# The row limits of two score tiles made in one VectorE operation instead of two

## The chip, the cores and the metric

The kernel runs on one core of a Trainium2 chip. The metric is the device time of one execution in microseconds (us). The core has TensorE (PE: matmuls, transposes), VectorE (DVE), ScalarE (ACT), GpSimd (POOL) and SyncE (SP, which issues the loads and moves here). Each engine works through its own queue in order; they meet at semaphores. TensorE's granted clock is 1.00 of its full level throughout.

## The reference

Attention over 4 batches of 8 heads with 576 rows and 64 features, followed by two MLP layers over 2304 tokens, all fp32. The part around the change:

```python
scores = scale * np.matmul(q, k.transpose(0, 1, 3, 2))
thresh = np.max(scores, axis=-1, keepdims=True) - tau
scores = np.where(scores >= thresh, scores, -1000000000.0)
scores = scores - np.max(scores, axis=-1, keepdims=True)
attn = np.exp(scores)
attn = attn / (np.sum(attn, axis=-1, keepdims=True) + 1e-09)
return np.matmul(attn, v).astype(np.float32)
...
h = x @ w_in
r = np.maximum(h, 0.0)
g = s * (r * r) + b
return (g @ w_out).astype(np.float32)
...
h = x @ w_in
g = h * (1.0 / (1.0 + np.exp(-1.702 * h)))
return (g @ w_out).astype(np.float32)
```

## The kernel before

The attention is cut into 160 tiles of 96 or 128 query rows by 576 keys. Two tiles, j even and j odd, make a beat; there are 80 beats with tiles and a few behind them. Matmul operands are split into a high and a low part of a narrower format (`_hi`, `_lo`, `q_hl`); ScalarE makes the high parts, GpSimd most of the low ones by a subtraction.

A tile goes through these steps. TensorE computes its scores into one of two PSUM tensors (`scores[j % 2]`). DVE's `row_max(j)` (L1045) multiplies them by the negative scale in place and writes the row's minimum, the negated maximum, to column `j % 8` of `neg_max`; this form comes as two instructions, the main one and a read of the accumulator (`DVE_READ_ACCUMULATOR`). ScalarE takes the exponent into `prob` (L1269). `limit_of(j)` (L1052) adds tau to that column of `neg_max` and writes the column of `limit`. `mask(j)` (L1071) zeroes what lies beyond the limit and sums the row. GpSimd adds epsilon to the two sums of a beat (L1547); `invert_pair` (L1059) on DVE takes their reciprocals in the next beat; GpSimd's norm (L1554) scales both tiles. TensorE and ScalarE turn the tiles of the first groups over, DVE (L1085) with moves by SyncE those of the later ones, and TensorE multiplies with the values: a context piece. ScalarE and DVE (`act_lo`, L1093) split a piece into high and low for the layers.

From beat 15 on (`MLP_FROM`) each beat also carries one step `s = beat - 15` of the first layer: on TensorE `output` of step s - 3 and `hidden` of step s, on ScalarE the relu, on DVE `gated(s - 1)` (L1101) and `gated_lo(s - 2)` (L1108, the tile `g_lo`), on GpSimd the low parts of two weight slabs (L1560, L1567). GpSimd's splits of a query tile (L1532) and a key tile (L1540) fall in the beats in which one is due.

The order on every engine is written out by hand in that engine's block. DVE's beat is: maximum and limit of the even tile, piece, reciprocals, gated, maximum and limit of the odd tile, mask of the even tile, g_lo, mask of the odd tile, piece, transposes. DVE's semaphore `max_ready` counts maxima, `limit_ready` limits. Before a tile's scores are overwritten, TensorE waits for the mask of the tile two before (`masked`).

Of the kernel before, what the change touches and what calls it, by code (L numbers as in the profile page):

```python
# [9 lines left out]
ALU = mybir.AluOpType  # L10
# [45 lines left out]
TILES = FIRST_TILE[-1]  # L56
# [11 lines left out]
def rows_of(j):  # L68
    return ROWS[GROUPS_OF[TILE_AT[j][0]][3]]
# [245 lines left out]
def tiles_of(beat, lag=0):  # L315
    return range(2 * beat - lag, 2 * beat - lag + 2)
# [41 lines left out]
def build(nc, q, k, v, consts_in, ident_in, slabs, twin_in, twin_out, out):  # L358
    ctx = ExitStack()
    with ctx:  # L360
# [7 lines left out]
        tau_in, s_c, b_c, eps_c, scale_c, tau_c, lower_c = (consts[:, n:n + 1] for n in range(7))  # L368
# [68 lines left out]
        neg_max = sbuf(attn, "neg_max", [P, STATS])  # L437
        limit = sbuf(attn, "limit", [P, STATS])
# [44 lines left out]
        max_ready = sem("max_ready")  # L483
        exp_ready = sem("exp_ready")
        limit_ready = sem("limit_ready")
# [532 lines left out]
        def _(dve):  # L1018
# [27 lines left out]
                                        accum_out=neg_max[0:m, j % STATS:j % STATS + 1]  # L1046
                                        ).then_inc(max_ready, 1)

            def limit_of(j):
                m, r = rows_of(j), j % STATS  # L1050
                dve.wait_ge(max_ready, j + 1)
                nc.vector.tensor_scalar(limit[0:m, r:r + 1], neg_max[0:m, r:r + 1], tau_c[0:m, :], None, ALU.add  # L1052
                                        ).then_inc(limit_ready, 1)

            def invert_pair(j):
# [5 lines left out]
            def mask(j):  # L1061

                m, r = rows_of(j), j % STATS
                dve.wait_ge(limit_ready, j + 1)
                dve.wait_ge(exp_ready, j + 1)
                if j % 2 == 1 and riding(j // 2) is not None:
                    dve.wait_ge(context_hi_ready, riding(j // 2) + 1)
                if j % 2 == 0 and turn_due(j // 2 - MLP_FROM) is not None:
                    dve.wait_ge(x_ready, turns_by(j // 2 - MLP_FROM))
                p = prob[0:m, j % PROBS, :].rearrange("p (a n) -> p a n", a=2)  # L1070
                nc.vector.scalar_tensor_tensor(  # L1071
                    out=p, in0=scores[j % 2][0:m, :, 0:HALF], scalar=limit[0:m, r:r + 1],
                    in1=p, op0=ALU.is_le, op1=ALU.mult,
                    accum_out=row_sum[0:m, r:r + 1]).then_inc(masked, 1)
# [22 lines left out]
            def gated(n):  # L1097

                dve.wait_ge(gate_ready, n + 1)
                g = gate[:, n % 2, :]  # L1100
                nc.vector.scalar_tensor_tensor(out=g, in0=h_bank(n)[:, 0:TOK], scalar=s_c, in1=g, op0=ALU.mult,  # L1101
                                               op1=ALU.mult).then_inc(square_ready, 1)
# [80 lines left out]
            for beat in range(BEATS):  # L1183
                s = beat - MLP_FROM
                for j in tiles_of(beat):
                    if j < TILES:
                        row_max(j)
                        limit_of(j)
                    if j % 2 == 0 and alone(beat - 1) is not None:
                        context_lo(alone(beat - 1))  # L1190
                    if j % 2 == 0 and 0 <= j - 2 < TILES:
                        invert_pair(j - 2)
                    if j % 2 == 0 and s >= 1:
                        gated(s - 1)
                for j in tiles_of(beat):
                    if j < TILES:
                        mask(j)
                    if j % 2 == 0 and s >= 2:
                        gated_lo(s - 2)
                if riding(beat) is not None:  # L1200
                    context_lo(riding(beat))
                for j in tiles_of(beat, 2):
                    if PE_TILES <= j < TILES:
                        turn(j)
# [497 lines left out]
```

## Time and profile before

| | |
|---|---|
| median of 3 runs | 1011.58 us (1011.28 to 1013.16) |
| the profiled execution | 1009.4 us, of which the span of the trace is 1007.6 us |
| TensorE busy | 993.2 us, 99% of the span |
| VectorE busy | 798.0 us, 79%, 1749 instructions |
| GpSimd busy | 657.9 us, 65% |
| ScalarE busy | 606.6 us, 60% |
| granted clock of TensorE | 1.00 |

Busy time counts an instruction from its start to the end that the profiler gives it; on TensorE the ends are modelled, and neighbours overlap, so 99% is not a peak rate. In a timeline an instruction's start is the more exact figure, and the step from start to start tells what an instruction cost its engine. DVE's busy time is spread unevenly: the attention ends at about 490 us.

### The profile page before, as it was taken

Reading aid. Unit: us, or ns where it says so; the run is one execution under the profiler, and the core shown is the slowest. Engines: PE = TensorE matmul, PEld = TensorE weight load, DVE = VectorE, ACT = ScalarE, POOL = GpSimd, SP = SyncE. Lnnn points to the kernel's source line nnn. Section 1 sums busy time; section 2 is a strip of 40 time slices with the busy share of each in tenths; the row PEclk is TensorE's granted clock in tenths of the full one; section 3 lists DMA queues with packets and bytes.
Section 4 is the critical chain, followed back from the end, with each engine's and each line's share of the span. In section 5 each row is a group of like instructions: output and inputs, shape, how many; then the busy total and the mean of one; then the engine's idle time right before and its main releaser. Section 6 shows DMA issues by size and latency. Waiting matters only on the chain.

```text
span 1007.6 us, 18212 instructions
## 1 busy us (share of the span) xinstructions
PE 993.2 (99%) x5922; PEld 895.4 (89%) x5922; DVE 798.0 (79%) x1749; ACT 606.6 (60%) x1124; POOL 657.9 (65%) x713
## 2 busy tenths in 40 slices
PE   8999999999999999999999999999999999999998
PEld 7788888888888888888899999998989989899897
DVE  7989999999999999999547766877767776566663
ACT  7877666666676666765555755555546555454443
POOL 6769997778788888886657775454544545445452
PEclk9999999999999999999999999999999999999999
DMA  7236776897977797778733541112122221222212
GB/s 216 73 116 187 209 204 189 218 239 213 228 199 191 204 246 190 209 179 217 211 106 126 185 150 32 63 42 85 44 82 87 102 84 46 81 87 102 84 48 79
DMA packets 97581, 142.50 MB, mean 141 GB/s; under 512 B 10320, under 2 KB 68944, under 8 KB 97488
## 3 DMA queue, kind: packets, MB, share of 16 engines
q1 hardware_dynamic: 97488, 141.34, 48.7%
q8 instruction: 49, 0.80, 0.3%
q14 instruction: 44, 0.36, 0.1%
HBM read 102.96 MB, written 4.72 MB: 107 GB/s over the span
## 4 chain that ended last, share of the span: by engine, by line
PE 85%; DVE 11%; issue 1%; DMA 1%; ACT 1%; POOL 0%; SPq 0%; DVEq 0%; POOLq 0%; ACTq 0%
PE shared L831 12%; PE y_ps L850 11%; PE shared L924 10%; PE y_ps L948 10%; PE scores L948 10%; PE scores L924 8%; PE scores L745 7%; PE scores L807 7%; PE scores L831 5%; PE y_ps L870 5%; DVE scores L1045 4%; DVE prob L1071 3%; PE scores L870 2%; DVE blocks L1085 1%; DMA k_raw<-k 1%
## 5 line engine op out<-in xcount | busy, mean ns | idle before, releaser
L1269 ACT ACTIVATE prob<-scores,neg_max 128x576 f32<-128x576 f32 (+1 forms) x160 | 118.6, 742 | 122.5 <-DVE scores L1045 122.4
L1614 POOL TENSOR_TENSOR a_sum_lo<-a_sum,a_hi 128x256 fp32r<-128x256 f32 x96 | 70.1, 740 | 182.5 <-DVE scores L1167 123.9
L1560 POOL TENSOR_TENSOR w_lo<-w_raw,win_hi 128x512 fp32r<-128x512 f32 x96 | 129.1, 1345 | 22.1 <-ACT win_hi L1311 17.7
L1567 POOL TENSOR_TENSOR w_lo<-w_raw,wout_hi 128x512 fp32r<-128x512 f32 x96 | 126.5, 1318 | 23.4 <-ACT wout_hi L1318 23.4
L1045 DVE TENSOR_SCALAR_CACHE_REDUCE scores<-scores,consts 128x576 f32<-128x576 f32 (+1 forms) x160 | 129.5, 809 | 13.1 <-PE scores L745 11.7
L1554 POOL TENSOR_SCALAR prob<-prob,row_inv 128x576 f32<-128x576 f32 (+1 forms) x160 | 126.8, 805 | 6.1 <-DVE row_inv L1059 5.7
L1071 DVE SCALAR_TENSOR_TENSOR prob<-scores,limit,prob 128x576 f32<-128x576 f32 (+1 forms) x160 | 128.1, 808 | 0.3
L831 PE MATMUL shared<-act_hi,win_hi 128*128 128x384 f32 x280 | 94.8, 339 | 1.1 <-DVE gate L1101 0.9
L831 PE MATMUL shared<-act_hi,w_lo 128*128 128x384 f32 x280 | 94.3, 337 | 0.0
L831 PE MATMUL shared<-act_lo,win_hi 128*128 128x384 f32 x280 | 93.9, 335 | 0.0
L1085 DVE STREAM_TRANSPOSE blocks<-prob 128x576 f32<-128x576 f32 (+1 forms) x128 | 91.4, 751 | 1.9 <-DMA prob_t<-blocks 1.7
L1108 DVE SCALAR_TENSOR_TENSOR g_lo<-gate,consts,g_hi 128x384 fp32r<-128x384 f32 x96 | 92.7, 966 | 0.2 <-ACT g_hi L1332 0.2
L1179 DVE TENSOR_TENSOR g_lo<-gate,g_hi 128x384 fp32r<-128x384 f32 x96 | 62.2, 650 | 33.4 <-ACT g_hi L1403 32.8
L745 PE MATMUL scores<-k_hi,q_hl 128*128 128x288 f32 (+1 forms) x320 | 76.6, 320 | 6.8 <-DVE prob L1071 6.2
L1332 ACT ACTIVATE g_hi<-gate,consts 128x384 fp32r<-128x384 f32 x96 | 59.0, 614 | 38.8 <-PE y_ps L870 27.9
L1395 ACT ACTIVATE gate<-scores 128x384 f32<-128x384 f32 x48 | 23.6, 492 | 94.9 <-DVE scores L1167 94.9
L1403 ACT CAST g_hi<-gate 128x384 fp32r<-128x384 f32 x96 | 49.2, 514 | 49.4 <-DVE gate L1174 40.0
L850 PE MATMUL y_ps<-wout_hi,g_hi 128*128 128x512 f32 x192 | 75.6, 394 | 0.0
L850 PE MATMUL y_ps<-wout_hi,g_lo 128*128 128x512 f32 x192 | 75.5, 393 | 0.0
L807 PE MATMUL scores<-prob_t,v_sb 128*64 128x192 f32 x800 | 73.8, 331 | 1.5 <-DVE prob L1071 0.9
L850 PE MATMUL y_ps<-w_lo,g_hi 128*128 128x512 f32 x192 | 74.9, 390 | 0.0
L1532 POOL TENSOR_TENSOR q_hl<-q_raw,q_hl 128x384 fp32r<-128x384 f32 (+1 forms) x51 | 49.0, 961 | 37.7 <-DVE g_lo L1108 31.2
(157 smaller groups left out, 2956.6 us busy)
## 6 DMA issues: line engine op xcount, KB each, us to landing
w_raw<-slabs SPq DMA_DIRECT2D x93, 512.0 KB, 4.2
a_raw<-twin_in SPq DMA_DIRECT2D x24, 512.0 KB, 4.6
o_raw<-twin_out SPq DMA_DIRECT2D x24, 512.0 KB, 3.6
prob_t<-blocks SPq DMA_DIRECT2D x96, 120.0 KB, 2.8
k_raw<-k SPq DMA_DIRECT2D x32, 288.0 KB, 4.6
prob_t<-blocks SPq DMA_DIRECT2D x96, 96.0 KB, 2.9
v_sb<-v SPq DMA_DIRECT2D x26, 320.0 KB, 4.3
q_raw<-q SPq DMA_DIRECT2D x40, 192.0 KB, 4.4
```

The lines of the kernel that those rows point to most:

```text
L745: mm = nc.tensor.matmul(scores[j % 2][0:m, half, 0:HALF], q_hl[i % Q_RING][:, q0:q0 + m], part[key_slot(e)][:, half * HALF:(half + 1) * HALF],
L807: mm = nc.tensor.matmul(place, v_sb[:, i % 2, side, c, :], rows, start=(c == 0), stop=(c == KEY_CHUNKS - 1))
L831: mm = nc.tensor.matmul(bank[:, 0:TOK], wp[:, w], act_at(xp, c, tile * TOK, TOK), start=(c == 0 and k == 0), stop=(c == DC - 1 and k == 2))
L850: mm = nc.tensor.matmul(y_ps[g][:], gp[:, n % 2, toks], wp[:, :], start=(f == 0 and k == 0), stop=(f == SLABS - 1 and k == 2))
L924: mm = nc.tensor.matmul(twin_bank(x), wp, xp, start=(c == 0 and k == 0), stop=(c == 1 and k == 2))
L948: mm = nc.tensor.matmul(z_bank(tile, g), gp[:, i, toks], wp, start=(e == 0 and i < 2 and k == 0), stop=(e == TWIN_SLABS - 1 and i >= 2 and ...
L1045: nc.vector.tensor_scalar(place, place, scale_c[0:m, :], None, ALU.mult, ALU.min, accum_out=neg_max[0:m, j % STATS:j % STATS + 1]).then_in ...
L1071: nc.vector.scalar_tensor_tensor(out=p, in0=scores[j % 2][0:m, :, 0:HALF], scalar=limit[0:m, r:r + 1], in1=p, op0=ALU.is_le, op1=ALU.mult, ...
L1269: nc.scalar.activation(prob[0:m, j % PROBS, :].rearrange("p (a n) -> p a n", a=2), scores[j % 2][0:m, :, 0:HALF], ACT.Exp, bias=neg_max[0: ...
L1554: nc.gpsimd.tensor_scalar(prob[0:m, j % PROBS, :], prob[0:m, j % PROBS, :], row_inv[0:m, r:r + 1], 1.0, ALU.mult, ALU.mult).then_inc(norme ...
L1560: nc.gpsimd.tensor_tensor(in_of(w_lo, n), in_of(w_raw, n), win_hi[n % IN_HI][:].bitcast(F32), ALU.subtract).then_inc(win_lo_ready, 1)
L1567: nc.gpsimd.tensor_tensor(out_of(w_lo, n), out_of(w_raw, n), wout_hi[n % OUT_HI][:].bitcast(F32), ALU.subtract).then_inc(wout_lo_ready, 1)
```

## The change

The limits of a beat's two tiles are no longer made one by one, each behind its own maximum. One operation with two columns makes both, behind the second maximum and ahead of the first mask. It waits for both maxima and counts `limit_ready` up by one for the two tiles; `mask` waits for the beat's count.

```diff
-            def limit_of(j):
+            def limit_pair(j):
+
                 m, r = rows_of(j), j % STATS
-                dve.wait_ge(max_ready, j + 1)
-                nc.vector.tensor_scalar(limit[0:m, r:r + 1], neg_max[0:m, r:r + 1], tau_c[0:m, :], None, ALU.add
+                dve.wait_ge(max_ready, j + 2)
+                nc.vector.tensor_scalar(limit[0:m, r:r + 2], neg_max[0:m, r:r + 2], tau_c[0:m, :], None, ALU.add
                                         ).then_inc(limit_ready, 1)
...
             def mask(j):
 
                 m, r = rows_of(j), j % STATS
-                dve.wait_ge(limit_ready, j + 1)
+                dve.wait_ge(limit_ready, j // 2 + 1)
                 dve.wait_ge(exp_ready, j + 1)
...
                 for j in tiles_of(beat):
                     if j < TILES:
                         row_max(j)
-                        limit_of(j)
                     if j % 2 == 0 and alone(beat - 1) is not None:
                         context_lo(alone(beat - 1))
                     if j % 2 == 0 and 0 <= j - 2 < TILES:
                         invert_pair(j - 2)
                     if j % 2 == 0 and s >= 1:
                         gated(s - 1)
+                if 2 * beat < TILES:
+                    limit_pair(2 * beat)
                 for j in tiles_of(beat):
                     if j < TILES:
                         mask(j)
```

No other engine's sequence changes. On VectorE, in a beat ahead of the first layer (a beat of 96-row tiles; scores0 and scores1 are the tensors of the even and the odd tile), the rows before are

```order
L1045 TENSOR_SCALAR scores0,neg_max<-scores0,consts 96x2x288 [waits scores_ready]
L1052 TENSOR_SCALAR limit<-neg_max,consts 96x1 [waits max_ready]
L1093 TENSOR_TENSOR act_lo0<-shared,act_hi0 128x128 [waits context_hi_ready]
L1059 RECIPROCAL row_inv<-row_sum_eps 128x2 [waits sum_eps_ready]
L1045 TENSOR_SCALAR scores1,neg_max<-scores1,consts 96x2x288 [waits scores_ready]
L1052 TENSOR_SCALAR limit<-neg_max,consts 96x1 [waits max_ready]
L1071 SCALAR_TENSOR_TENSOR prob,row_sum<-scores0,limit,prob 96x576 [waits exp_ready,limit_ready]
```

and of the changed kernel, same engine and place:

```order
L1045 TENSOR_SCALAR scores0,neg_max<-scores0,consts 96x2x288 [waits scores_ready]
L1094 TENSOR_TENSOR act_lo0<-shared,act_hi0 128x128 [waits context_hi_ready]
L1060 RECIPROCAL row_inv<-row_sum_eps 128x2 [waits sum_eps_ready]
L1045 TENSOR_SCALAR scores1,neg_max<-scores1,consts 96x2x288 [waits scores_ready]
L1053 TENSOR_SCALAR limit<-neg_max,consts 96x2 [waits max_ready]
L1072 SCALAR_TENSOR_TENSOR prob,row_sum<-scores0,limit,prob 96x576 [waits exp_ready,limit_ready]
```

The first limit is gone, the second has two columns, and the first mask needs the result of the operation directly ahead of it. (From L1053 on the changed kernel's lines have numbers higher by one.)

On VectorE in a beat with a layer step, where `gated` (gate<-shared) stands between the two maxima, the rows before are

```order
L1045 TENSOR_SCALAR scores0,neg_max<-scores0,consts 96x2x288
L1052 TENSOR_SCALAR limit<-neg_max,consts 96x1
L1059 RECIPROCAL row_inv<-row_sum_eps 128x2
L1101 SCALAR_TENSOR_TENSOR gate<-shared,consts,gate 128x384
L1045 TENSOR_SCALAR scores1,neg_max<-scores1,consts 96x2x288
```

and of the changed kernel:

```order
L1045 TENSOR_SCALAR scores0,neg_max<-scores0,consts 96x2x288
L1060 RECIPROCAL row_inv<-row_sum_eps 128x2
L1102 SCALAR_TENSOR_TENSOR gate<-shared,consts,gate 128x384
L1045 TENSOR_SCALAR scores1,neg_max<-scores1,consts 96x2x288
L1053 TENSOR_SCALAR limit<-neg_max,consts 96x2
```

The reciprocals and `gated` come directly behind the first maximum.

## Rows read from the trace of the kernel before

**Rows 1.** The page's part 1, busy time, share and instructions by engine.

```profile
PE 993.2 (99%) x5922; PEld 895.4 (89%) x5922; DVE 798.0 (79%) x1749; ACT 606.6 (60%) x1124; POOL 657.9 (65%) x713
```

**Rows 2.** Three stretches: length, busy PE, PEld, DVE, ACT, POOL; clock, DMA share, GB/s.

```profile
10.00:66.00 56.00, 49.79 (x496) 43.49 (x496) 52.83 (x164) 46.80 (x96) 41.30 (x61) 1.00 0.36 112
66.00:132.00 66.00, 63.44 (x406) 55.88 (x404) 63.31 (x164) 48.28 (x94) 60.65 (x66) 1.00 0.66 195
132.00:484.00 352.00, 351.40 (x2262) 309.43 (x2261) 337.23 (x846) 230.92 (x432) 284.37 (x322) 1.00 0.80 209
```

**Rows 3.** Waits of DVE from 132 to 484 us: total, times, longest.

```profile
DVE scores L1045 <- PE scores L745: 8.8, 19, 1.1
DVE blocks L1085 <- DMA prob_t<-blocks: 1.7, 3, 0.9
```

**Rows 4.** The chain that ended last, in beat 9: start, us, what.

```profile
43.90 0.21 DVE limit L1052
...
46.21 0.81 PE scores L745 x4
```

**Rows 5.** Timeline of DVE, beat 9: start us, us, instruction, idle before.

```profile
42.98 0.83 DVE L1045 TENSOR_SCALAR_CACHE_REDUCE scores<-scores,consts 128x576 f32<-128x576 f32 x1 [0.15 <-PE scores L745]
43.72 0.14 DVE L1045 DVE_READ_ACCUMULATOR scores<-scores,consts 128x1 f32 x1
43.90 0.21 DVE L1052 TENSOR_SCALAR limit<-neg_max,consts 128x1 f32<-128x1 f32 x1
44.03 0.28 DVE L1093 TENSOR_TENSOR act_lo<-shared,act_hi 128x128 fp32r<-128x128 f32 x1
44.23 0.15 DVE L1059 RECIPROCAL row_inv<-row_sum_eps 128x2 f32<-128x2 f32 x1
...
45.20 0.21 DVE L1052 TENSOR_SCALAR limit<-neg_max,consts 128x1 f32<-128x1 f32 x1
45.34 0.81 DVE L1071 SCALAR_TENSOR_TENSOR prob<-scores,limit,prob 128x576 f32<-128x576 f32 x1
46.07 0.08 DVE L1071 DVE_READ_ACCUMULATOR prob<-scores,limit,prob 128x1 f32 x1
46.07 0.81 DVE L1071 SCALAR_TENSOR_TENSOR prob<-scores,limit,prob 128x576 f32<-128x576 f32 x1
```

**Rows 6.** Timeline of DVE, three of the second layer's weight sums.

```profile
591.27 0.41 DVE L1149 TENSOR_TENSOR a_sum<-a_raw 128x256 f32<-128x256 f32 x1
591.60 0.41 DVE L1151 TENSOR_TENSOR a_sum<-a_raw,a_sum 128x256 f32<-128x256 f32 x1
592.05 1.41 DVE L1154 TENSOR_TENSOR a_sum<-a_raw,a_sum 128x256 f32<-128x256 f32 x1
```

**Rows 7.** Three lines of DVE: duration in ns, least/median/greatest; first and last start.

```profile
L1052 DVE TENSOR_SCALAR limit<-neg_max,consts x160: 208/214/217, 7.9 to 481.2; 128x1 f32<-128x1 f32 x96, 96x1 f32<-96x1 f32 x64
...
L1059 DVE RECIPROCAL row_inv<-row_sum_eps x80: 119/154/158, 11.8 to 484.9; 128x2 f32<-128x2 f32 x80
...
L1108 DVE SCALAR_TENSOR_TENSOR g_lo<-gate,consts,g_hi x96: 607/617/1728, 81.0 to 627.4; 128x384 fp32r<-128x384 f32 x96
```

**Rows 8.** Timeline of POOL in beats 2, 9, 10 and 22.

```profile
16.41 1.40 POOL L1540 TENSOR_TENSOR k_lo<-k_raw,k_hi 128x576 fp32r<-128x576 f32 x1
...
44.48 1.47 POOL L1554 TENSOR_SCALAR prob<-prob,row_inv 128x576 f32<-128x576 f32 x2 [0.41 <-DVE row_inv L1059]
...
48.54 1.47 POOL L1554 TENSOR_SCALAR prob<-prob,row_inv 128x576 f32<-128x576 f32 x2
...
110.63 1.78 POOL L1554 TENSOR_SCALAR prob<-prob,row_inv 96x576 f32<-96x576 f32 x2
```

**Rows 9.** Timeline of DVE: the second limit in beats 2, 10 and 22.

```profile
16.88 0.21 DVE L1052 TENSOR_SCALAR limit<-neg_max,consts 128x1 f32<-128x1 f32 x1
...
49.26 0.21 DVE L1052 TENSOR_SCALAR limit<-neg_max,consts 128x1 f32<-128x1 f32 x1
...
111.02 0.21 DVE L1052 TENSOR_SCALAR limit<-neg_max,consts 96x1 f32<-96x1 f32 x1
```

## The prediction

> **What bounds the kernel now.** I read the page's busy shares first: TensorE (PE) is busy 993.2 us of the 1007.6 us span, VectorE (DVE) 798.0 [rows 1]. An average over stages says little, so next came the busy time by stretch. The reader is to see three regimes in it [rows 2]. In 10 to 66 us (attention alone, beats 1 to 14) DVE is busy 52.8 of 56 us and PE 49.8. In 66 to 132 us (the first layer joins) DVE has 63.3 of 66, PE 63.4, GpSimd (POOL) 60.7. In 132 to 484 us PE has 351.4 of 352 and DVE 337.2. Third, the waits of DVE in that last stretch: 8.8 us for PE's scores and 1.7 us for a move, 10.5 us in 54 beats [rows 3]. So DVE sets the pace up to about 132 us, and behind that PE does, with DVE some 0.2 us a beat from setting it.
>
> The chain shows the loop of an early beat: first limit 0.21 us, and at the end the first mask's result lets PE compute the next scores, 0.81 us [rows 4], which the next first maximum waits for. The two maxima, the limits and the first mask are all inside; only the second mask lies beside the scores. What a beat saves or loses ahead of its first mask is therefore lost or won in full up to 66 us.
>
> **The change, step by step.** All steps below are start-to-start times of one early beat [rows 5].
>
> Removed: the first limit and its wait. The first maximum's accumulator read starts at 43.72, the limit that waits for it at 43.90 (0.18), and the next instruction, which waits for neither, at 44.03 (0.13). Where nothing waits on an accumulator read, the next instruction starts with it: behind the first mask, read and second mask both start at 46.07. Taking that for the maximum too, act_lo starts at 43.72 instead of 44.03: 0.31 us less. Bounds: if the maximum's read of 0.14 us can't be overlapped, 0.17 is left.
>
> Added: the first mask now waits for an operation that stands directly before it. At 45.20 the limit starts and the mask follows at 45.34, since it waits only for the limit of long before. The nearest rows are three sums: the second (591.60) starts 0.33 behind its predecessor, whose result it doesn't need, and the third, which waits for the second, 0.45 behind that one [rows 6]. So a wait on the predecessor costs 0.12. I take 0.12, bounds 0.05 (the mask's issue hides a part) and 0.18 (the step from read to limit). Second column: reciprocal with two columns is shorter than limit with one, 154 against 214 ns [rows 7], so I give it nothing. Net so far: 0.31 less, 0.12 more, 0.19 us a beat less, between 0 and 0.26.
>
> On that price the Trainium skill says otherwise: "VectorE: DVE Perf Modes", section "The DRAIN you can't avoid", has a chain of Vector operations take the same time with a semaphore behind each as with one at the end, and advises fewer operations, not fewer waits. By that rule only the limit's own step of 0.13 would be saved and no 0.12 added, 0.13 a beat less instead of 0.19. Rows 5 and 6 disagree with it: the waits there cost 0.18 and 0.12.
>
> The term that decides is what the new operation meets. In the old form limit lasts 208 to 217 ns in all 160 cases though GpSimd is nearly always at work; reciprocal is as constant; but g_lo lasts from 607 to 1728 ns, by what GpSimd runs beside it [rows 7]. So there are DVE operations that GpSimd's hold up, for up to 1.1 us, and others that it doesn't. A tensor-with-scalar operation from SBUF to SBUF that is more than one column wide has no row in this trace. Bounds: nothing, as for one column, or the rest of the GpSimd instruction in progress. I take the second, by choice: the two free rows are one of the old width and one of another operation.
>
> The Trainium skill is what tips me. "SBUF — State Buffer", section "Who interferes with whom", has tensor_scalar (not the form with an accumulator) enter modes that use both port pairs, and then it and GpSimd exclude each other for a whole instruction; "Vector Engine (DVE) Microarchitecture Reference", section 5.1, has fp32 with two elements per partition do so. g_lo in rows 7 agrees in kind; the two-column limit no run here shows.
>
> Price of it: the pair arrives where the second limit starts now, less 0.31. Let POOL's instruction in progress run to its end, and add 0.1 for handing over (of the size of the 0.12 above). Beats 1 to 14 fall in three kinds.
> - Six (1, 5, 8, 9, 11, 13): the norms are released by reciprocal and move with it. The first norm (44.48, now 44.17, 0.74 long) ends at 44.91, and the pair comes at 44.89 [rows 5, 8]. Wait 0.02, net 0.17 less: together 1.0 less.
> - Three (10, 12, 14): a wider q split ahead keeps the norms back. Norm from 48.54 to 49.28, pair at 48.95 [rows 8, 9]. Wait 0.43, net 0.24 more: 0.7 more.
> - Five (2, 3, 4, 6, 7): the 1.40 us split of a key runs. In beat 2 it lasts from 16.41 to 17.8, and the pair comes at 16.57 [rows 8, 9]: 1.3. The five waits read 1.3, 1.0, 0.6, 0.6, 0.6, sum 4.2, less 5 x 0.19: 3.2 more.
>
> Sum to 66 us: 2.9 us slower. Beats 15 and 16 wait for the first matmuls of the layer and count nothing. Beats 17 to 25 read the same way give waits from 0 to 0.76 (beat 22: norm from 110.63, pair at 110.71 instead of 111.02, 0.65 and 0.1 [rows 8, 9]), in sum 4.3, less 9 x 0.19: 2.6 slower; POOL, as full as DVE there, can't give it back. Beats 26 to 79: waits 22.7 us in 54 beats, less 54 x 0.19: 12.4 us more on DVE, against 10.5 us that it waits now. PE hides most; about 1 us is left. What is late next, if the cover is gone, is the masks: behind the pair stand both masks, g_lo and the transposes, and PE's next scores wait for the masks. Bounds: 0 and, with half a wait more in each beat, 6.
>
> Sum: 2.9 + 2.6 + 1 = 6.5 us. The profiled execution took 1009.4 us, so 1015.9 by its measure; the median of the three runs is 2.2 us above it. Forecast: 1018.0 us.
>
> **The rivals.**
> - *Held by nothing, faster.* The pair starts at once beside any GpSimd instruction, as limit and reciprocal do [rows 7]. Then 14 x 0.19 = 2.7 us up to 66 us. From 66 to 132 us DVE would save 9 x 0.19 = 1.7, but PE idles only 2.6 us there [rows 2] and POOL is near full; I give 1.0. Behind that PE is the bound: 0. Together 3.7: 1007.9 us. For it: 160 steady limits. Against it: nothing but the width. It decides once the mean wait is under 0.19 us a beat.
> - *The accumulator read isn't overlapped.* The saving is 0.17, the new wait 0.12 to 0.18: 0.05 or 0 a beat, at most 14 x 0.05 = 0.7 us: 1011.3 us. For it: the maximum's read lasts 0.14, the mask's 0.08. Against it: the mask's read is wholly overlapped.
> - *Held, but the wait falls away.* The key splits are fed by ScalarE and the masks of the beat before, so that the beat could settle with the pair between two instructions, as six beats do already: waits of 0.2 a beat on average, no difference: 1011.6 us. Against it: the two instructions that follow on POOL stand in its queue with no gap.
>
> **How the numbers follow.** Chances: forecast mechanism 0.60 (nearly all of it slower), held by nothing 0.25, read not overlapped 0.07, wait falls away 0.08. A measurement of this kernel tells about 0.2%, 2.0 us. Slower: 0.60 less 0.04 for a size under 2 us = 0.56; faster: 0.25 less 0.03 = 0.22; the rest, 0.22, within. The range starts below the rival's 1007.9, since it holds a quarter, at 1007.2 and ends at 1022.0, where late beats leak 4 to 5 us instead of 1. The forecast's own range is 1014 to 1022.
>
> **What would show it.** Right: the new limit lasts from 0.21 up to 1.5 us, or the gap behind the maximum's read grows, case by case with POOL's instruction; 80 of them hold 20 to 35 us; the norms in turn stretch; the beats of the first kind shrink by 0.1 to 0.2 us, and the ones with a key split grow by 0.4 or more. DVE's wait for PE in 132 to 484 us goes towards 0. The step maximum to act_lo is 0.74 instead of 1.05, and pair to mask 0.25 where POOL is idle. Wrong: 80 limits of 0.21 to 0.22 us. Then the first rival holds, and every early beat shrinks by 0.19 us; if its act_lo starts 0.14 later than the read, the second.

## The result and the profile of the changed kernel

The changed kernel takes 1019.03 us in the median of six runs (1017.29 to 1020.27), the kernel before 1010.63 us in six (1009.16 to 1013.16). The ratio is 1.0088, with a 95% interval of 1.0076 to 1.0099: slower by 0.9%. The profiled execution of the changed kernel took 1018.54 us, its span is 1016.7 us, 9.1 us more than before.

The page's part 1 of the changed kernel, which answers to [rows 1]:

```profile
span 1016.7 us, 18132 instructions
PE 994.8 (98%) x5922; PEld 895.9 (88%) x5922; DVE 805.0 (79%) x1669; ACT 609.4 (60%) x1124; POOL 655.7 (64%) x713
```

DVE has 80 instructions fewer and is busy 7.0 us longer. The same three stretches as in [rows 2]:

```profile
10.00:66.00 56.00, 46.80 (x454) 41.45 (x456) 51.62 (x138) 43.09 (x87) 38.48 (x57) 0.97 0.35 108
66.00:132.00 66.00, 62.23 (x418) 53.72 (x415) 63.32 (x152) 48.85 (x95) 56.81 (x64) 1.00 0.64 186
132.00:484.00 352.00, 348.77 (x2236) 307.09 (x2235) 336.35 (x787) 231.22 (x430) 284.15 (x321) 1.00 0.78 206
```

PE does 3.0 us less of its work up to 66 us, 1.2 less up to 132 and 2.6 less up to 484, so all three stretches lose.

Two lines of DVE, durations in ns least/median/greatest, against [rows 7]. First the new limit:

```profile
L1053 DVE TENSOR_SCALAR limit<-neg_max,consts x80: 223/555/830, 8.9 to 489.7; 128x2 f32<-128x2 f32 x48, 96x2 f32<-96x2 f32 x32
...
L1060 DVE RECIPROCAL row_inv<-row_sum_eps x80: 119/158/168, 11.6 to 494.0; 128x2 f32<-128x2 f32 x80
```

The old limit took 208 to 217 ns in 160 cases. The new one takes from 223 to 830 ns. By its two shapes, busy time and mean of one:

```profile
L1053 DVE TENSOR_SCALAR limit<-neg_max,consts 128x2 f32<-128x2 f32 x48 | 22.8, 475 | 1.7
...
L1053 DVE TENSOR_SCALAR limit<-neg_max,consts 96x2 f32<-96x2 f32 x32 | 17.9, 559 | 1.1
```

That is 40.7 us in all; 80 free ones of 0.225 us would be 18.0. So they take 22.7 us more than free ones would. This is what being held means below; 62 of the 80 last over 0.24 us. The reciprocal, of two columns as well, stays nearly as it was (158 ns in the middle, 154 before).

What holds it is seen where the timelines of DVE and of POOL are laid side by side. DVE in beat 9, against [rows 5]:

```profile
45.87 0.83 DVE L1045 TENSOR_SCALAR_CACHE_REDUCE scores<-scores,consts 128x576 f32<-128x576 f32 x1 [0.15 <-PE scores L745]
46.61 0.14 DVE L1045 DVE_READ_ACCUMULATOR scores<-scores,consts 128x1 f32 x1
46.61 0.29 DVE L1094 TENSOR_TENSOR act_lo<-shared,act_hi 128x128 fp32r<-128x128 f32 x1
46.82 0.15 DVE L1060 RECIPROCAL row_inv<-row_sum_eps 128x2 f32<-128x2 f32 x1
46.95 0.83 DVE L1045 TENSOR_SCALAR_CACHE_REDUCE scores<-scores,consts 128x576 f32<-128x576 f32 x1
47.69 0.14 DVE L1045 DVE_READ_ACCUMULATOR scores<-scores,consts 128x1 f32 x1
47.87 0.69 DVE L1053 TENSOR_SCALAR limit<-neg_max,consts 128x2 f32<-128x2 f32 x1
48.60 0.82 DVE L1072 SCALAR_TENSOR_TENSOR prob<-scores,limit,prob 128x576 f32<-128x576 f32 x1
```

And POOL, against [rows 8]:

```profile
47.07 1.47 POOL L1556 TENSOR_SCALAR prob<-prob,row_inv 128x576 f32<-128x576 f32 x2 [0.39 <-DVE row_inv L1060]
```

The two norms run from 47.07 to 48.54, so the second starts at 47.80. The limit is issued at 47.87, into that second norm, and ends at 48.56, 0.02 us behind it. In this trace 61 of the 62 end 0.02 to 0.03 us behind the end of a GpSimd instruction (norm L1556, k_lo L1542 or w_lo L1569); the other one, in beat 30, lasts only 0.25 us.

That also gives the price. A pair (the new limit of two columns) that starts with the time t to go in GpSimd's instruction lasts t + 0.02 us where t is over 0.2, and 0.23 us where it is less: its own 0.23 us run beside the wait and not behind it. So it costs t less 0.2. Beat 7 lies close to that limit: the pair starts 0.25 us before the end of a key split and lasts 0.27 us, hardly more than a free one. DVE first, then POOL:

```profile
39.41 0.27 DVE L1053 TENSOR_SCALAR limit<-neg_max,consts 128x2 f32<-128x2 f32 x1
...
38.24 1.41 POOL L1542 TENSOR_TENSOR k_lo<-k_raw,k_hi 128x576 fp32r<-128x576 f32 x1
```

All 56 pairs with more than 0.25 us to go follow this. Of the pairs that come within 0.04 us of the end of one instruction, those of beats 1 and 14 are free, and those of beats 21, 24, 42 and 75 are held to the end of the next (0.75 to 0.79 us).

From the first maximum to the first mask beat 9 took 2.36 us before (42.98 to 45.34 in [rows 5]) and takes 2.73 now. The beat grew nearly as much, from 4.06 to 4.45 us. This step from first maximum to first mask, called the **head** of a beat below, is the number by which the experiments are compared; all heads are of beat 8 or 9, which are alike in each kernel.

DVE's waits from 132 to 484 us, against [rows 3]; the wait for the move is gone, the one for PE is not:

```profile
DVE scores L1045 <- PE scores L745: 11.4, 19, 1.1
```

The chain that ended last, shares by engine: PE holds 76% (85% before), DVE 16% (11%).

```profile
PE 76%; DVE 16%; DMA 3%; issue 2%; ACT 2%; SPq 1%; POOL 0%; DVEq 0%; POOLq 0%; ACTq 0%
```

GpSimd has 0% in it. It has no share, although the experiments below show that it causes the delay: no semaphore joins it to the limit, and a held instruction shows up as a long instruction of the engine that is held.

### The profile page after: what moved, and what is told of

The parts are those of the page before. It is cut to its first block, busy times and chain, and to the rows that moved or that the text cites. A ratio compares the mean times of both kernels' runs of the same rounds, so it can differ in the third digit from the quotient of the medians.

```text
span 1016.7 us, 18132 instructions
## 1 busy us (share of the span) xinstructions
PE 994.8 (98%) x5922; PEld 895.9 (88%) x5922; DVE 805.0 (79%) x1669; ACT 609.4 (60%) x1124; POOL 655.7 (64%) x713
## 4 chain that ended last, share of the span: by engine, by line
PE 76%; DVE 16%; DMA 3%; issue 2%; ACT 2%; SPq 1%; POOL 0%; DVEq 0%; POOLq 0%; ACTq 0%
PE shared L924 10%; PE scores L948 10%; PE y_ps L948 10%; PE shared L831 8%; PE scores L924 8%; PE y_ps L850 7%; PE scores L807 6%; DVE scores L1045 5%; PE scores L745 5%; PE scores L831 5%; PE y_ps L870 5%; DVE prob L1072 3%; DVE blocks L1086 3%; DVE g_lo L1109 2%; PE scores L870 2%
## 5 line engine op out<-in xcount | busy, mean ns | idle before, releaser
L1569 POOL TENSOR_TENSOR w_lo<-w_raw,wout_hi 128x512 fp32r<-128x512 f32 x96 | 126.5, 1318 | 23.5 <-ACT wout_hi L1320 23.5
L1556 POOL TENSOR_SCALAR prob<-prob,row_inv 128x576 f32<-128x576 f32 (+1 forms) x160 | 124.9, 794 | 3.6 <-DVE row_inv L1060 3.3
L1109 DVE SCALAR_TENSOR_TENSOR g_lo<-gate,consts,g_hi 128x384 fp32r<-128x384 f32 x96 | 88.7, 924 | 0.2 <-ACT g_hi L1334 0.2
L807 PE MATMUL scores<-prob_t,v_sb 128*64 128x192 f32 x800 | 73.8, 331 | 4.4 <-DVE prob L1072 4.3
```

The source lines that it names most:

```text
L807: mm = nc.tensor.matmul(place, v_sb[:, i % 2, side, c, :], rows, start=(c == 0), stop=(c == KEY_CHUNKS - 1))
L1556: nc.gpsimd.tensor_scalar(prob[0:m, j % PROBS, :], prob[0:m, j % PROBS, :], row_inv[0:m, r:r + 1], 1.0, ALU.mult, ALU.mult).then_inc(norme ...
L1569: nc.gpsimd.tensor_tensor(out_of(w_lo, n), out_of(w_raw, n), wout_hi[n % OUT_HI][:].bitcast(F32), ALU.subtract).then_inc(wout_lo_ready, 1)
```

## The experiments

Each edit is against the kernel before or the changed kernel, as said. The ratio is to the kernel before, run beside it (medians from 1010.14 to 1010.53 us), with its 95% interval. The theory under test: two columns make the limit wait out GpSimd's instruction in progress. The rivals: the loss is the new wait of the mask on its predecessor, or the order alone.

### The order alone, with narrow limits

From the kernel before: both limits behind the second maximum, each of one column.

```diff
                         row_max(j)
-                        limit_of(j)
...
                 for j in tiles_of(beat):
+                    if j < TILES:
+                        limit_of(j)
+                for j in tiles_of(beat):
                     if j < TILES:
                         mask(j)
```

> The order of the change without its width: both limits one column wide, directly behind each other after the second maximum. Theory (the two-column form is held by GpSimd's instructions): all 160 limits last 0.21 to 0.22 us, none follows GpSimd. The first beats save the first limit's wait (0.18 us) and nothing else; the second mask's wait lies behind the first mask: 14 x 0.18 = 2.5 us up to 66 us, about 1 us behind that, so 3 us faster than before (ratio 0.997). Rival (the order is what costs: the masks come later because the limits stand together): about as slow as the change, ratio 1.006 to 1.009.

Measured: 1005.56 us, ratio 0.9960 (0.9945 to 0.9974): faster. DVE in beat 9; x2 is the two limits together:

```profile
42.21 0.83 DVE L1045 TENSOR_SCALAR_CACHE_REDUCE scores<-scores,consts 128x576 f32<-128x576 f32 x1 [0.16 <-PE scores L745]
...
44.02 0.14 DVE L1045 DVE_READ_ACCUMULATOR scores<-scores,consts 128x1 f32 x1
44.02 0.39 DVE L1052 TENSOR_SCALAR limit<-neg_max,consts 128x1 f32<-128x1 f32 x2
44.33 0.81 DVE L1071 SCALAR_TENSOR_TENSOR prob<-scores,limit,prob 128x576 f32<-128x576 f32 x1
```

And all 160 limits, durations in ns as above:

```profile
L1052 DVE TENSOR_SCALAR limit<-neg_max,consts x160: 197/210/216, 8.8 to 476.7; 128x1 f32<-128x1 f32 x96, 96x1 f32<-96x1 f32 x64
```

The head is 2.12 us, 0.24 less than before, and no limit is held, though they stand in the place of the pair and 96 of the 160 start with more than 0.25 us to go in a GpSimd instruction. The first limit starts together with the second maximum's read, since it needs only the first maximum, and the first mask needs only the first limit. So the rival of the order is refuted: the place isn't what costs, and with two narrow limits it is a gain.

### The wait alone

From the kernel before: the mask of the even tile also waits for the odd tile's limit, which stands directly ahead of it.

```diff
-                dve.wait_ge(limit_ready, j + 1)
+                dve.wait_ge(limit_ready, j - j % 2 + 2)
```

> The order and both one-column limits of before; only the masks wait for both limits of their beat, so that the first mask waits for the operation directly before it. It prices the wait that the change adds. Both theories: pair-to-mask step 0.24 to 0.26 instead of 0.14 us, 14 x 0.12 = 1.7 us more up to 66 us and up to 9 x 0.12 = 1 us more from 66 to 132 us; ratio 1.001 to 1.003. If the wait is the main cost of the change, the ratio is 1.006 or more.

Measured: 1013.32 us, ratio 1.0031 (1.0018 to 1.0044).

```profile
46.17 0.21 DVE L1052 TENSOR_SCALAR limit<-neg_max,consts 128x1 f32<-128x1 f32 x1
46.42 0.82 DVE L1071 SCALAR_TENSOR_TENSOR prob<-scores,limit,prob 128x576 f32<-128x576 f32 x1
```

The step from limit to mask is 0.25 us, against 0.14 in [rows 5]; the head grows from 2.36 to 2.47 and the early beats from 4.05 to 4.18. So the wait costs 0.11 us an early beat here, and in all about a third of what the change lost.

The Trainium skill, "VectorE: DVE Perf Modes", "The DRAIN you can't avoid", has a chain of eight copies take the same time with a semaphore behind each as with one at the end. This run weighs against carrying that over to this kernel: the wait is the only edit, and the time moved.

### The width alone, on top of the wait

From the kernel with the wait alone: the odd tile's limit writes both columns. Even tiles keep their own narrow limit, so the count of instructions, the order and the waits don't change.

```diff
+                first = r - j % 2
-                nc.vector.tensor_scalar(limit[0:m, r:r + 1], neg_max[0:m, r:r + 1], tau_c[0:m, :], None, ALU.add
+                nc.vector.tensor_scalar(limit[0:m, first:r + 1], neg_max[0:m, first:r + 1], tau_c[0:m, :], None, ALU.add
```

> As the run with the wait alone, and the second limit of a beat makes both columns again, two wide; the first limit stays. The two kernels differ in the width of 80 operations. Theory (held by width): the 80 wide limits last 0.22 to 1.5 us by what GpSimd runs, the 80 narrow ones 0.21; slower than the change itself, since the first limit and its wait are still there: ratio 1.010 to 1.020. Rival (width costs nothing): the same as the run with the wait alone.

Measured: 1020.46 us, ratio 1.0110 (1.0094 to 1.0127). Wide and narrow limits of the one kernel, busy time and mean of one:

```profile
L1053 DVE TENSOR_SCALAR limit<-neg_max,consts 128x2 f32<-128x2 f32 x48 | 17.8, 371 | 1.7
...
L1053 DVE TENSOR_SCALAR limit<-neg_max,consts 96x2 f32<-96x2 f32 x32 | 13.8, 431 | 1.1
...
L1053 DVE TENSOR_SCALAR limit<-neg_max,consts 128x1 f32<-128x1 f32 x48 | 10.3, 214 | 1.7
...
L1053 DVE TENSOR_SCALAR limit<-neg_max,consts 96x1 f32<-96x1 f32 x32 | 6.7, 209 | 1.1
```

This is the cleanest pair: 80 operations are one column wider, and the median is 7.1 us longer (1020.46 less 1013.32). The granted clock doesn't explain it: the mean of an execution is 0.997 or 0.998 in three of the four with the wide limit, but the fourth, at 1.000, still took 1019.89 us. Where it costs differs from the changed kernel. Here nearly all the early beats are free (4.20 us, against 4.18 with the wait alone): in beat 9 the reciprocal starts at 46.07 and the wide limit at 47.04, 0.97 behind it, and the first norm runs from 46.32 to 47.06, so the limit finds 0.02 us to go and lasts 0.23. Only beat 2 is clearly longer (4.82 us, 3.98 with the wait alone). In the changed kernel it comes 1.05 behind the reciprocal and waits for nearly the whole second norm. The loss lies behind: the start of beat 14 is 0.9 us later than with the wait alone, of beat 26 1.9 and of beat 79 6.5.

### The changed kernel with an accumulating pair

From the changed kernel: the pair gets an accumulator output that nobody reads; the two columns are computed as they were.

```diff
+        unused = sbuf(attn, "unused", [P, STATS])
...
-                nc.vector.tensor_scalar(limit[0:m, r:r + 2], neg_max[0:m, r:r + 2], tau_c[0:m, :], None, ALU.add
-                                        ).then_inc(limit_ready, 1)
+                nc.vector.tensor_scalar(limit[0:m, r:r + 2], neg_max[0:m, r:r + 2], tau_c[0:m, :], None, ALU.add,
+                                        ALU.min, accum_out=unused[0:m, r:r + 1]).then_inc(limit_ready, 1)
```

> The changed kernel with its two-column operation in the form that also writes an accumulator (the least of the two limits, to a column nobody reads). Same place, same width, same waits, another form. Theory (the plain form takes a port pair that GpSimd holds, the accumulating one doesn't): 80 limits of constant length, about 0.2 us plus an accumulator read of 0.14; the mask then waits 0.14 to 0.2 longer than for a free plain one. Early beats about as long as before, ratio 0.996 to 1.001. Rival (any two-column operation there is held): ratio 1.008 to 1.012.

Measured: 1008.59 us, ratio 0.9983 (0.9973 to 0.9994).

```profile
L1054 DVE TENSOR_SCALAR_CACHE_REDUCE limit<-neg_max,consts x80: 209/215/217, 9.2 to 480.0; 128x2 f32<-128x2 f32 x48, 96x2 f32<-96x2 f32 x32
```

Same place, same columns, same waits, one instruction more (the read of the accumulator), and none of 80 is held, though 50 of them start with more than 0.25 us to go in a GpSimd instruction. Beat 9 is a case, the pair of DVE and the norms of POOL, the first of which ends at about 45.08 and the second at 45.81:

```profile
45.14 0.21 DVE L1054 TENSOR_SCALAR_CACHE_REDUCE limit<-neg_max,consts 128x2 f32<-128x2 f32 x1
...
44.34 1.47 POOL L1557 TENSOR_SCALAR prob<-prob,row_inv 128x576 f32<-128x576 f32 x2 [0.26 <-DVE row_inv L1061]
```

The changed kernel's loss is gone, by another form of the same operation. The head is 2.26 us, the regular early beats 3.97. The longer step to the mask that was expected for the accumulator's read didn't come. This is the change as the first rival of the prediction imagined it, and its gain is 0.17%, not the 3.7 us (0.37%) that the rival was given.

The Trainium skill, "SBUF — State Buffer", "Who interferes with whom", excludes the accumulating form from the modes in which VectorE and GpSimd exclude each other. This run and the one above agree: 0 of 80 held with the accumulator, 62 of 80 without in the changed kernel.

### The norms cut down, in both kernels

In the changed kernel and in the kernel before, GpSimd's norm works on one column instead of 576; the weights stay unnormalised. The work behind it is otherwise the same.

```diff
-                nc.gpsimd.tensor_scalar(prob[0:m, j % PROBS, :], prob[0:m, j % PROBS, :], row_inv[0:m, r:r + 1],
+                nc.gpsimd.tensor_scalar(prob[0:m, j % PROBS, 0:1], prob[0:m, j % PROBS, 0:1], row_inv[0:m, r:r + 1],
                                         1.0, ALU.mult, ALU.mult).then_inc(normed, 1)
```

> The changed kernel with GpSimd's norm cut to one column of each tile, so that the weights stay unnormalised; every semaphore is as it was. Theory (the two-column limit is held for as long as the GpSimd instruction beside it runs): in the early beats that have no key split beside the pair its length falls from 0.70 to 0.23 us, since only the norm held it there; held limits are left where splits of slabs and keys run. The 80 limits sum to 22 to 30 us instead of 40.7. Against the same cut in the kernel before: 0 to 4 us faster or at most 1 slower. Rival (the hold comes from the order of the maxima, or from a wait): the limits stay at about 0.5 us each.

> The kernel before with the same cut of GpSimd's norm to one column. It is what the run of the changed kernel with that cut is compared with. Both theories: the early beats, paced by VectorE, stay at 4.05 us; GpSimd idles 1.4 us a beat more; g_lo is held less often from 66 to 132 us, so that up to 2 us may go: ratio 0.997 to 1.000.

Measured: changed 1008.77 us, ratio 0.9979 (0.9969 to 0.9988); before 1007.99 us, ratio 0.9973 (0.9961 to 0.9985). Without the norms the two kernels can't be told apart: their intervals overlap nearly whole. The pair of the changed one:

```profile
L1053 DVE TENSOR_SCALAR limit<-neg_max,consts x80: 223/228/803, 8.8 to 479.5; 128x2 f32<-128x2 f32 x48, 96x2 f32<-96x2 f32 x32
```

DVE in its beat 9:

```profile
42.87 0.83 DVE L1045 TENSOR_SCALAR_CACHE_REDUCE scores<-scores,consts 128x576 f32<-128x576 f32 x1
43.61 0.14 DVE L1045 DVE_READ_ACCUMULATOR scores<-scores,consts 128x1 f32 x1
43.61 0.28 DVE L1094 TENSOR_TENSOR act_lo<-shared,act_hi 128x128 fp32r<-128x128 f32 x1
43.82 0.15 DVE L1060 RECIPROCAL row_inv<-row_sum_eps 128x2 f32<-128x2 f32 x1
43.94 0.83 DVE L1045 TENSOR_SCALAR_CACHE_REDUCE scores<-scores,consts 128x576 f32<-128x576 f32 x1
44.68 0.14 DVE L1045 DVE_READ_ACCUMULATOR scores<-scores,consts 128x1 f32 x1
44.86 0.23 DVE L1053 TENSOR_SCALAR limit<-neg_max,consts 128x2 f32<-128x2 f32 x1
45.12 0.82 DVE L1072 SCALAR_TENSOR_TENSOR prob<-scores,limit,prob 128x576 f32<-128x576 f32 x1
```

The norm is what held most of the pairs: the sum of the 80 falls from 40.7 to 22.4 us, of which 4.4 is still over 80 free ones; 17 pairs still last over 0.24 us, 15 of them up to the end of a low split of GpSimd. The head is 2.25, 0.11 less than before the change. That is what the change gives an early beat where nothing holds it.

### The limits spread out, and the first limit moved alone

From the kernel before: the even limit behind `gated`, still ahead of the second maximum, and the odd limit behind the even tile's mask. Both are one column wide. Neither stands directly behind the maximum that it needs, and none is left between the second maximum and the first mask. The odd tile's mask, beside the scores, now waits for the limit directly ahead of it in an early beat.

```diff
                         row_max(j)
-                        limit_of(j)
...
                         gated(s - 1)
+                    if j % 2 == 0 and j < TILES:
+                        limit_of(j)
                 for j in tiles_of(beat):
                     if j < TILES:
                         mask(j)
+                    if j % 2 == 0 and j < TILES:
+                        limit_of(j + 1)
```

> Both limits one column wide and each behind an operation that isn't its source: the even tile's behind the reciprocals and the gated product, the odd tile's behind the first mask. No limit waits for the maximum directly ahead of it. Theory (waits of 0.18 us on the maximum and the place ahead of the first mask are what the limits cost): the first mask of an early beat comes 0.3 us or more sooner than before, the second waits for its limit beside the scores; early beats 3.7 us, 14 x 0.35 = 5 us up to 66 us and 1 to 2 behind it: ratio 0.993 to 0.995, under the run with two narrow limits behind the second maximum (0.996). Rival (TensorE, ScalarE or GpSimd paces an early beat as soon as VectorE needs less than about 3.85 us): ratio 0.996, the same as that run.

Measured: 1004.43 us (1004.13 to 1006.06), ratio 0.9938 (0.9924 to 0.9953), the fastest version here.

```profile
42.52 0.82 DVE L1045 TENSOR_SCALAR_CACHE_REDUCE scores<-scores,consts 128x576 f32<-128x576 f32 x1
...
43.53 0.19 DVE L1052 TENSOR_SCALAR limit<-neg_max,consts 128x1 f32<-128x1 f32 x1
43.64 0.82 DVE L1045 TENSOR_SCALAR_CACHE_REDUCE scores<-scores,consts 128x576 f32<-128x576 f32 x1
44.38 0.14 DVE L1045 DVE_READ_ACCUMULATOR scores<-scores,consts 128x1 f32 x1
44.38 0.81 DVE L1071 SCALAR_TENSOR_TENSOR prob<-scores,limit,prob 128x576 f32<-128x576 f32 x1
```

The first mask now starts with the second maximum's read: the head is 1.86 us. With the even limit moved and the odd one left where it was:

```diff
                         row_max(j)
-                        limit_of(j)
+                        if j % 2 == 1:
+                            limit_of(j)
...
                         gated(s - 1)
+                    if j % 2 == 0 and j < TILES:
+                        limit_of(j)
```

> Half of the spread: only the even tile's limit moves behind the reciprocals and the gated product; the odd tile's stays behind its maximum with its wait. Theory: the first limit's wait of 0.18 us goes and nothing else changes: early beats 3.87 us, ratio 0.996 to 0.998. Rival as for the full spread: the same.

Measured: 1007.26 us, ratio 0.9963 (0.9950 to 0.9976), head 2.17 us. So 0.19 of the 0.50 us come from the even limit and 0.31 from the odd one. The early beats follow where a key split isn't due: 4.06 us before, 3.87 with the even limit moved, 3.62 with both, where the odd one gives 0.25 of its 0.31.

### TensorE kept busier at the start

The changed kernel's beat 3 lasts 5.17 us instead of the 4.4 of its neighbours, and its granted clock falls there. In the changed kernel:

```profile
18.00:22.00 4.00, 3.48 (x20) 3.08 (x22) 3.27 (x10) 2.45 (x6) 3.75 (x6) 0.73 0.95 316
20.00:21.00 1.00, 1.00 (x7) 0.98 (x6) 0.46 (x4) 0.72 (x1) 1.00 (x2) 0.50 0.99 397
```

In the 1 us from 20 us it is 0.50, the lower level of 1.2 GHz; before the fall TensorE had waited 2.0 us for a mask of DVE. The kernel has a table of repeated transposes that fill TensorE's early gaps; one more entry was added, to the changed kernel and to the spread one.

```diff
-AWAKE = (0, 8, 0, 7)
+AWAKE = (0, 8, 0, 7, 0, 6)
```

> The changed kernel with six idle matmuls of 128 columns (0.11 us each) behind the scores of tile 5, in the gap of TensorE at 15 to 17 us after which its granted clock stood at 0.50 for 4 us in the profile of the changed kernel. Theory (the held limits lengthen the loop, and the clock's fall is a small extra of one beat): the fall is gone, beat 3 goes from 5.17 to about 4.45 us, 0.7 to 1 us of the 8.4 comes back: ratio 1.007 to 1.008, limits held as before. Rival (the clock is a large part of the slowdown): ratio 1.005 or less.

> The spread limits with the same six idle matmuls. In the profile of the spread kernel the granted clock stood at 0.50 from 18.6 to 22 us, and beats 2 to 4 took 4.36 us instead of 3.6 to 3.9. Theory: the fall is gone and up to 1 us comes back: ratio 0.992 to 0.994. Rival (ScalarE and GpSimd pace those beats anyway): the same ratio as without, 0.9938.

Measured: changed 1017.67 us, ratio 1.0072 (1.0048 to 1.0097); spread 1005.37 us, ratio 0.9948 (0.9932 to 0.9963). Windows of the changed one:

```profile
18.00:22.00 4.00, 3.67 (x38) 3.23 (x38) 3.62 (x11) 3.99 (x9) 3.28 (x5) 1.00 0.94 301
```

The clock stays at 1.00 there and beat 3 lasts 4.46 us, but the median is only 1.4 us lower, and the interval overlaps with the change's own. In the spread kernel's profiled execution the clock fell all the same, earlier (0.71 from 14 to 18 us), and nothing was gained. The mean clock of each execution says more: that one took 1007.39 us at 0.998, the six others 1004.40 to 1005.46 at 1.000. Of the changed kernel's six executions two were at 1.000, and they took 1017.29 and 1019.21 us, inside the range of all. So the fall costs it some 0.7 us by beat 3 and 1.4 by the medians, out of 8.4: a side effect. Whether the held limits brought it about is left open. It came in four of the changed kernel's six executions and in none with the accumulating pair, but also in one of the spread kernel's and some of the kernel before's, which have no held limit.

### The norms told to wait for the pair

In the changed kernel GpSimd's norms wait for the pair of their beat, so that it can't fall into one.

```diff
+                if 1 <= beat <= TILES // 2 - 1:
+                    pool.wait_ge(limit_ready, beat + 1)
                 for j in tiles_of(beat, 2):
```

> The changed kernel with GpSimd's norms waiting for the two-column limit of the same beat, so that the limit finds no norm in progress. Theory (the hold is the norm's or the split's run time): limits 0.23 us in the early beats and wherever no slab or key split runs; but norms start some 0.8 us later in each beat, and the transposes on TensorE or VectorE that wait for them follow. Early beats 3.95 to 4.1 us; behind 66 us GpSimd, which is nearly full, waits in its queue and slabs come later: ratio 1.000 to 1.010 overall, with the first 66 us back at or under the length of before. Rival (the hold isn't the norm's): limits of 0.7 us in the early beats as before.

Measured: 1018.06 us, ratio 1.0072 (1.0045 to 1.0099): no gain that can be told. The pair, and behind it an early beat's norms, now released by the pair:

```profile
L1053 DVE TENSOR_SCALAR limit<-neg_max,consts x80: 223/228/1045, 8.6 to 489.3; 128x2 f32<-128x2 f32 x48, 96x2 f32<-96x2 f32 x32
```

```profile
44.08 1.47 POOL L1556 TENSOR_SCALAR prob<-prob,row_inv 128x576 f32<-128x576 f32 x2 [1.40 <-DVE limit L1053]
```

The sum of the limits fell from 40.7 to 28.5 us (20 are left over 0.24 us, each up to the end of a low split) and the regular early beats from 4.45 to 3.98 us, as wanted. But GpSimd waited 61.9 us for the pairs, and the rest of its queue moved back with the norms; beat 14 starts at 65.52 us, against 63.15 before and 67.98 in the changed kernel, with beats 2 and 3 at 6.38 and 4.93 us, where the granted clock fell again (0.63 from 18 to 22 us). Beat 79 starts at 487.00, against 487.36 in the changed kernel. The hold was traded for a wait of the other engine.

## Why the prediction held, point by point

The forecast was 1018.0 us, slower, and 1019.03 us were measured: the direction and the mechanism are right. That the two numbers lie only 1.0 us apart is in part luck. The forecast added 6.5 us to a median of 1011.58; the same kernel takes 1010.63 in six executions, so that 8.4 us were to be forecast. And the 6.5 us are a sum of errors of both signs, as the points below show: each hold was priced too high, and the place at which the pair arrives was read wrong in the other direction.

**The deciding term, "the rest of the GpSimd instruction in progress", is shown.** The duration goes with width (narrow 209 and 214 ns, wide 371 and 431 in one kernel), with the form (215 ns with the accumulator) and with what GpSimd does (228 ns median without the norms). The forecast was 80 limits from 0.21 to 1.5 us, holding 20 to 35 us; measured were 0.22 to 0.83 us and 22.7 us. The greatest of 1.5 didn't come: beat 2's pair met the key split with 0.69 us to go instead of 1.3, and the longest of all, beat 40's, lasted 0.83. One sign failed: the norms were to stretch in turn, but the 160 are busy 124.9 us, against 126.8 before.

**"Add 0.1 for handing over" is wrong in sign.** A held pair costs the time to go less 0.2 us, as shown above, where the prediction took the time to go plus 0.1: 0.3 us too much for each pair that is held. Its six beats of the first kind are counted without their own 0.1, at a wait of 0.02; by its own rule they would have given 0.07 less each and not 0.17, and a sum of about 3.5 us in place of 2.9. (The five waits at key splits add up to 4.1 as listed, not 4.2.)

**"0.31 less", the removed limit and its wait:** the step maximum to act_lo is 0.74 (45.87 to 46.61) instead of 1.05. Right.

**"0.12 more", the wait on the predecessor:** 0.11 to 0.12, limit to mask 0.26 where nothing holds it and 0.25 with the wait alone. Right.

**"Net 0.19 us a beat less" is wrong in size.** Unheld, the head shrinks by 0.11 (2.36 to 2.25) or 0.10 (2.26 with the accumulator), and the beats by 0.08 to 0.1. The missing 0.08 lies in steps that I counted as unchanged: from reciprocal to second limit it was 0.97 us in [rows 5], and 1.05 in the changed kernel (46.82 to 47.87). Most of it is the step from reciprocal to second maximum: 0.07 in both runs that keep the limit ahead of act_lo and change only the waits or the width, 0.12 or 0.13 in the changed kernel and the five runs that take it away and leave the reciprocal directly ahead of the maximum. It isn't so in every beat: in the changed kernel's beats 7 and 14 the step is 0.07 again (38.44 to 38.51, 68.93 to 69.00). Why it is so isn't shown.

**The three kinds of early beats: the sum was too small and its parts were wrong.**
- First kind (1, 5, 8, 9, 11, 13), predicted 0.17 less each. The margin was 0.02 us: a first norm that ends 0.99 us behind the reciprocal and a pair that comes 0.97 behind it. The pair came 1.05 behind the reciprocal, 0.07 into the *second* norm, and was held to its end, which costs 0.47 us. In the run with the wait and the width, where it did come 0.97 behind the reciprocal, it was free. Five of the six went from between 4.01 and 4.06 us to between 4.40 and 4.45 (beat 1 stayed, at 4.08), in sum 1.95 us more, where 1.0 less was forecast. This is the step that failed: the wait rises and falls like a sawtooth with the time of arrival, and it was read at one point, 0.02 us from the edge.
- Second kind (10, 12, 14), predicted 0.24 more each; measured 0.39 more in beats 10 and 12 and 0.23 less in beat 14, in sum 0.55 instead of 0.7.
- Key splits (2, 3, 4, 6, 7), predicted 3.2 us more; measured 2.0, of which 1.2 are beat 3, where the clock fell. In beat 2 the pair met the split with 0.69 us to go, in beats 6 and 7 with 0.20 and 0.25. In beats 3 and 4 it met the first norm behind it (pair from 21.72 to 22.28, norms from 21.51), while beats 6 and 7 stayed near their length, at 3.97 and 4.09 us. The pair of beat 6 on DVE:

```profile
35.35 0.23 DVE L1053 TENSOR_SCALAR limit<-neg_max,consts 128x2 f32<-128x2 f32 x1
```

POOL beside it:

```profile
34.14 1.41 POOL L1542 TENSOR_TENSOR k_lo<-k_raw,k_hi 128x576 fp32r<-128x576 f32 x1
35.53 1.49 POOL L1556 TENSOR_SCALAR prob<-prob,row_inv 128x576 f32<-128x576 f32 x2
```

The pair came at the tail of the split and just ahead of the norms. That is the rival "held, but the wait falls away", true for these two beats and not for the kernel.

**The stages.** The start of a beat against before, from the first maxima: beat 14 starts 4.8 us later (67.98 against 63.15), beat 26 5.9 (139.92 against 133.98), beat 79 8.8 (487.36 against 478.56). So the three stages cost 4.8, 1.1 and 2.9 us, where 2.9, 2.6 and 1 were forecast; 0.3 more lies behind, in sum 9.1 of span against 6.5. (Beat 14 itself, 0.23 us shorter, falls into the second stage here.) The middle was too high. The late one was too low, for two errors that work against each other. The holds there are 13.3 us instead of 22.7, so that, by an estimate with 0.1 us saved in each of 54 beats, DVE has about 8 us more to do and not 12.4. But 2.9 us of them reached the end instead of 1: I hid most behind DVE's 10.5 us of waiting. The bounds of 0 to 6 hold the result.

**"DVE's wait for PE goes towards 0" is wrong.** It rose from 8.8 to 11.4 us, with the wait for the move gone. DVE's idle time there isn't a store from which holds are paid. PE waits more for the masks in that stretch, in its weight loads for the matmuls with the values (L807), first the changed kernel and then the one before:

```profile
PEld scores L807 <- DVE prob L1072: 6.5, 15, 0.8
...
PEld scores L807 <- DVE prob L1071: 1.9, 8, 0.4
```

So a held pair delays the masks, and PE behind them. That DVE's own wait for the next scores follows from this fits the rows and isn't shown by a run of its own.

**The first rival, "held by nothing", is refuted in its mechanism and also in its price.** The run in which no pair is held, with the accumulator, gains 0.17% (0.06 to 0.27%). Where both kernels have their norms cut the change gains nothing, with 4.4 us of holds left in it. I gave 3.7 us, with the net of 0.19 and with gains behind 66 us that aren't there. "The accumulator read isn't overlapped" is refuted by the step of 0.74.

## What to carry to other kernels

Merging two small VectorE operations into one can change more than their count: if the merged form is a `tensor_scalar` of two fp32 columns from SBUF to SBUF, without an accumulator, budget each time for what is left of the GpSimd instruction in progress, less the time that the operation takes anyway (0.2 us here), and read GpSimd's timeline at the moment when it comes. Wider ones weren't tried here. Where the expected wait is a sawtooth of an engine's instructions, price both sides of the edge, not the point. An operation of 0.2 us is best taken off the path that paces the beat and away from the operation whose result it needs, which gave 0.6% here with no operation saved, while saving 80 of them lost 0.9%.

## What was not expected of the hardware

- The cost of a one-column operation on this path is mostly where it stands: from between the maximum and its follower to behind the reciprocal, the even limit saves 0.19 us a beat (head 2.36 to 2.17), and the odd one behind the mask another 0.31, while each limit still takes about 0.2 us.
- An accumulator output that nobody needs takes the pair out of GpSimd's way: 215 ns in 80 of 80 cases, and its own read of 82 ns costs nothing: from pair to mask it is 0.26 us (45.14 to 45.40), as with the plain form.
- What is left of GpSimd's instruction is free up to 0.2 us. The pair of beat 6 starts at 35.35, while the key split of GpSimd has 0.20 us to go, lasts 0.23 us like a free one, and ends 0.03 us behind the split, as the long holds do. Whether the pair does nothing until GpSimd is done, or only its end waits, this trace doesn't tell.
